# Softmax reciprocals stored as one row per head pair, and a new order of work where attention ends

## What is computed

```python
attn = np.exp(scores)
attn = attn / (np.sum(attn, axis=-1, keepdims=True) + 1e-09)
x = np.matmul(attn, v).transpose(0, 2, 1, 3).reshape(B * S, H * D)
h = x @ w_in
x = np.where(h > 0.0, h, np.exp(np.minimum(h, 0.0)) - 1.0) @ w_out
# then, per token: x + gate * (relu(x @ w1[e]) @ w2[e]) for its expert e, where x @ w_skip > 0
```

## Time and profile before

| | us |
|---|---|
| median of 3 runs | 791.72 |
| lowest and highest run | 790.86, 791.75 |
| the profiled execution | 791.72 |
| its span | 789.9 |

### The profile page before, as it was taken

How to read it: one execution, slowest core, us unless ns; L and a number is a source line. 1 busy time by engine, 2 the same in 40 slices (tenths; PEclk the granted TensorE clock), 3 DMA queues, 4 the chain that set the end, 5 groups by cost and what they waited for, 6 DMA issues and landing times.

```text
span 789.9 us, 15565 instructions
## 1 busy us (share of the span) xinstructions
PE 758.0 (96%) x5170; PEld 639.8 (81%) x5171; DVE 524.1 (66%) x1331; ACT 347.8 (44%) x830; POOL 245.3 (31%) x240
## 2 busy tenths in 40 slices
PE   5999999899999999999999999999987999999995
PEld 3777777688998888898988998888865777887884
DVE  3888888954337974984797598436665997367342
ACT  3888888644322213223222322324452774446231
POOL 4888887944501201210121021000112231222211
PEclk9999999999999999999999999999998999999998
DMA  9556677462422112101210200502424898174000
GB/s 163 133 149 157 163 162 188 144 198 61 147 79 103 48 57 91 50 21 62 59 41 0 90 22 27 214 0 81 135 95 126 270 340 303 46 229 153 34 15 9
DMA packets 101061, 88.15 MB, mean 112 GB/s; under 512 B 63812, under 2 KB 78532, under 8 KB 100880
## 3 DMA queue, kind: packets, MB, share of 16 engines
q1 hardware_dynamic: 95584, 81.89, 34.7%
q0 software_dynamic: 3056, 5.00, 1.9%
q10 hardware_dynamic: 2368, 0.59, 0.4%
HBM read 72.26 MB, written 18.34 MB: 115 GB/s over the span
## 4 chain that ended last, share of the span: by engine, by line
PE 86%; ACT 5%; DVE 4%; issue 3%; DVEq 1%; DMA 1%; POOL 0%; SPq 0%; ACTq 0%; POOLq 0%
PE h_ps L1733 12%; PE out_ps L1733 12%; PE h_ps L1734 12%; PE h_ps L1735 12%; PE out_ps L1735 11%; PE out_ps L1734 11%; PE o_ps L684 5%; PE s_ps L668 3%; ACT prob L541 3%; PE t_ps L593 2%; PE out_ps L1869 1%; PE s_ps L663 1%; ACT pt L525 1%; PE tr_ps L1834 1%; DMA raw_qk<-in_q_dram 1%
## 5 line engine op out<-in xcount | busy, mean ns | idle before, releaser
L1558 ACT ACTIVATE ex<-h_ps 128x384 f32<-128x384 f32 x96 | 47.3, 493 | 272.3 <-PE h_ps L1735 272.3
L1733 PE MATMUL h_ps<-xt_hi,wi_hi 128*128 128x384 f32 x384 | 131.8, 343 | 0.0
L1734 PE MATMUL h_ps<-xt_lo,wi_hi 128*128 128x384 f32 x384 | 129.7, 338 | 0.0
L1735 PE MATMUL h_ps<-xt_hi,wi_lo 128*128 128x384 f32 x384 | 129.7, 338 | 0.0
L1394 DVE TENSOR_SCALAR ex<-ex 128x384 f32<-128x384 f32 x96 | 36.9, 385 | 131.1 <-ACT ex L1558 129.7
L1733 PE MATMUL out_ps<-wo_hi,gt 128*128 128x512 f32 x288 | 114.5, 398 | 0.0
L1735 PE MATMUL out_ps<-wo_hi,gt 128*128 128x512 f32 x288 | 113.9, 396 | 0.0
L1734 PE MATMUL out_ps<-wo_lo,gt 128*128 128x512 f32 x288 | 113.3, 393 | 0.0
L541 ACT ACTIVATE prob<-s_ps,negmax 128x128 f32<-128x128 f32 (+2 forms) x144 | 77.8, 556 | 14.1 <-DVE negmax L399 13.7
L1276 DVE CUSTOM_DVE_ANT_0 x2t<-x,w_raw 128x512 bf16<-128x512 f32 x108 | 82.7, 806 | 0.4
L1172 POOL TENSOR_TENSOR xt_lo<-x_raw,xt_hi 128x384 fp32r<-128x384 f32 x20 | 28.3, 1413 | 157.8 <-ACT xt_hi L1575 157.5
(11 more groups left out here) (180 smaller groups left out, 1589.0 us busy)
## 6 DMA issues: line engine op xcount, KB each, us to landing
w_raw<-in_moe_w_dram SPq DMA_DIRECT2D x56, 512.0 KB, 5.2
raw_qk<-in_q_dram SPq DMA_DIRECT2D x32, 144.0 KB, 3.2
attn_t<-attn_sb SPq DMA_DIRECT2D x16, 288.0 KB, 2.2
x_raw<-attn_t SPq DMA_DIRECT2D x24, 192.0 KB, 2.4
w_raw<-recip_rows SPq DMA_DIRECT2D x48, 96.0 KB, 2.8
out_dram<-x SPq DMA_DIRECT2D x18, 256.0 KB, 2.1
x_rows<-x SPq DMA_DIRECT2D x18, 256.0 KB, 2.6
v<-in_v_dram SPq DMA_DIRECT2D x32, 128.0 KB, 2.9
```

The source lines that it names most:

```text
L1558: act.activation(ex[:, f % 2], h_ps[:, f % 2, 0:NB], ACT.Exp).then_inc(ex_done, 1)
L1733: pe.matmul(dst, stat[0], mov[0], start=start, stop=False, skip_group_check=True)
L1734: pe.matmul(dst, stat[0], mov[1], start=False, stop=False, skip_group_check=True)
L1735: return pe.matmul(dst, stat[1], mov[0], start=False, stop=stop, skip_group_check=True)
```

## The change

The table becomes 16 rows of 1152 numbers, one row for each pair, and a pair is stored with one DMA (`store_recips`). A block of 384 tokens no longer lies in one piece of that table: per batch the first 512 tokens and the last 64 are apart, for each of the two heads. A new generator gives the pieces, and `load_recips` issues a DMA for each: 2 for a tile of blocks 0 and 3, 6 for one of blocks 1 and 4 (widths 128, 64 and 192 for each half), 4 for one of blocks 2 and 5. The semaphore counts follow.

Further, the reciprocals of block 1 are loaded by `load_r(1, k)`, after the x tiles of block 1 and ahead of the gates and w_out's chunks 8 to 15. The x tile 3 of block 0 and its reciprocals are loaded one step later. At the end of attention SP stores the reciprocals of pair 15 ahead of the result of pair 14, DVE copies the result of pair 14 after its reciprocals of pair 15, and PE does `values(14)` after `turn_mixed` and `turn_recips(15)` ahead of hidden(1).

```diff
+def recip_row(r_rows, b, k):
+    PAIR_TOKENS, MAIN = 576, 512
+    for batch in range(4):
+        first = batch * PAIR_TOKENS
+        for a, z, at in ((0, MAIN, 0), (MAIN, PAIR_TOKENS, 2 * MAIN)):
+            lo, hi = max(first + a, b * X_TILES * P), min(first + z, (b + 1) * X_TILES * P)
+            if lo < hi:
+                for h in range(2):
+                    col = at + h * (z - a) + lo - first - a
+                    yield (slice(h * P // 2, (h + 1) * P // 2), slice(lo - b * X_TILES * P, hi - b * X_TILES * P),
+                           r_rows[4 * batch + k:4 * batch + k + 1, col:col + hi - lo]
+                           .broadcast_to([P // 2, hi - lo]))
...
+    for rows, cols, src in recip_row(r_rows, b, k):
+        sp.dma_start(dst[rows, cols], src).then_inc(x_r_in[min(b, 2)][k], 16)
...
         def store_recips(n, i):
             wait(sp, r_row_done, n + 1)
-            rows, first = bass.ds((n % GROUP) * 2, 2), (n // GROUP) * S
-            sp.dma_start(r_all[rows, bass.ds(first, FULL * P)].rearrange("h (u q) -> h u q", q=P),
-                         r_rows[0:2 * FULL, :]).then_inc(r_stored, 16)
-            sp.dma_start(r_all[rows, bass.ds(first + FULL * P, TAIL)].rearrange("(o h) q -> o h q", o=1),
-                         r_rows[2 * FULL:COLS, :].rearrange("o (h q) -> o h q", h=2)).then_inc(r_stored, 16)
+            sp.dma_start(r_all[bass.ds(n, 1)].rearrange("o (c q) -> (o c) q", q=P), r_rows[:, :])\
+              .then_inc(r_stored, 16)
...
-            for c in ((0, 1), (2, 3), (), ())[m - PAIRS + 4]:
+            for c in {PAIRS - 4: (0, 1), PAIRS - 3: (2,), PAIRS - 2: (3,), PAIRS - 1: ()}[m]:
                 load_x_rows(sp, attn_t, c, 0, x_raw, x_in)
                 load_recips(sp, r_all, 0, c, x_r[0][c], x_r_in)
-            for c in ((), (), (0, 1), (2, 3))[m - PAIRS + 4]:
-                load_recips(sp, r_all, 1, c, x_r[1][c], x_r_in)
         sp.wait_ge(s_done, SCORES * (PAIRS - 1))
         first_wo()
+        store_recips(PAIRS - 1, 1)
         store(PAIRS - 2, 0)
-        store_recips(PAIRS - 1, 1)
         next_wo()
         store(PAIRS - 1, 1)
...
-            if older and not now:
-                final(*older)
             if past:
                 recips(past[0])
...
-            if older and now:
+            if older:
                 final(*older)
...
-        values(*older, (t1_out, PAIRS))
         turn_tile(PAIRS - 1, 3, t_ps, t3_done, (exp_done, exps(PAIRS - 1, 3, 1)), (t2_out, PAIRS))
         pe.wait_ge(wi_lo_done, PAIRS)
         hidden(0)
         pe.wait_ge(t3_out, PAIRS)
         turn_mixed(last, None)
+        values(*older, (t1_out, PAIRS))
+        turn_recips(PAIRS - 1)
         hidden(1)
-        turn_recips(PAIRS - 1)
         values(*last, (corner_out, PAIRS), (t3_out, PAIRS))
...
             load_x(1)
+            for k in range(KC):
+                load_r(1, k)
             load_gates()
             for f in range(2 * WR, FC):
                 load_wo(f)
```

More of the change, by code:

```diff
@@ L64, in attention, with recip_loads, normalise @@
     given.update(q=q, k=k, v=v, w_in=w_in)
-def load_recips(sp, r_rows, b, k, dst, x_r_in):
[L70 to L76, removed]
+def recip_row(r_rows, b, k):
[10 more added lines that the diff above has]
+                           .broadcast_to([P // 2, hi - lo]))
+def load_recips(sp, r_rows, b, k, dst, x_r_in):
+    for rows, cols, src in recip_row(r_rows, b, k):
+        sp.dma_start(dst[rows, cols], src).then_inc(x_r_in[min(b, 2)][k], 16)
+def recip_loads(r_rows, b, k):
+    return sum(1 for b1 in range(min(b, 2), b + 1) for _ in recip_row(r_rows, b1, k))
+def normalise(dve, x, r, x_in, x_r_in, x_norm, b, k, loads):
     dve.wait_ge(x_in[k], 16 * (b + 1))
-    dve.wait_ge(x_r_in[min(b, 2)][k], 32 * (max(b, 2) - 1))
+    dve.wait_ge(x_r_in[min(b, 2)][k], 16 * loads)
     dve.tensor_tensor(x[k][:, :], x[k][:, :], r, ALU.mult).then_inc(x_norm, 1)
@@ L315, in sync @@
             sp.wait_ge(stored[i], 16 * (GROUP // 2))
-        sp.wait_ge(r_stored, 32 * 2 * GROUP)
+        sp.wait_ge(r_stored, 16 * GROUP)
         for m in range(PAIRS - 4, PAIRS):
             step(m // 2, m % 2)
-            for c in ((0, 1), (2, 3), (), ())[m - PAIRS + 4]:
+            for c in {PAIRS - 4: (0, 1), PAIRS - 3: (2,), PAIRS - 2: (3,), PAIRS - 1: ()}[m]:
                 load_x_rows(sp, attn_t, c, 0, x_raw, x_in)
                 load_recips(sp, r_all, 0, c, x_r[0][c], x_r_in)
-            for c in ((), (), (0, 1), (2, 3))[m - PAIRS + 4]:
-                load_recips(sp, r_all, 1, c, x_r[1][c], x_r_in)
         sp.wait_ge(s_done, SCORES * (PAIRS - 1))
         first_wo()
+        store_recips(PAIRS - 1, 1)
         store(PAIRS - 2, 0)
-        store_recips(PAIRS - 1, 1)
         next_wo()
@@ L433, in recip_rows @@
             wait(dve, r_turned, n + 1)
-            wait(dve, r_stored, 32 * n)
+            wait(dve, r_stored, 16 * n)
             dve.tensor_copy(r_rows[:, :].rearrange("c (s w) -> c s w", s=2), t_ps[0:COLS, :, 0:D])\
@@ L493, in vector @@
             for c in {PAIRS - 2: (0, 1), PAIRS - 1: (2, 3), PAIRS: ()}[m]:
-                normalise(dve, x_raw, x_r[0][c], x_in, x_r_in, x_norm, 0, c)
+                normalise(dve, x_raw, x_r[0][c], x_in, x_r_in, x_norm, 0, c, recip_loads(r_all, 0, c))
             step(m // 2, m % 2)
@@ L802, in experts @@
         x_hi_done, x_lo_done = sem("x_hi_done"), sem("x_lo_done")
-        r_all = nc.dram_tensor("recip_rows", (2 * KC, N), F32, kind="Internal").ap()
+        r_all = nc.dram_tensor("recip_rows", (N // (TB * P) * 8 // 3, 9 * P), F32, kind="Internal").ap()
         x_r_in, x_norm = [[sem(f"x_r_in{b}_{k}") for k in range(KC)] for b in range(3)], sem("x_norm")
@@ L1039, in load_r @@
             def load_r(b, k):
-                if (b, k) > (2, 0):
+                if b > 1 and (b, k) > (2, 0):
                     sp.wait_ge(x_norm, KC * b + k)
@@ L1094, in _ @@
                 sp.wait_ge(stored, 16 * attend["pairs"] // 2)
-            sp.wait_ge(attend["r_stored"], 32 * attend["pairs"])
+            sp.wait_ge(attend["r_stored"], 16 * attend["pairs"])
             load_x(1)
+            for k in range(KC):
+                load_r(1, k)
             load_gates()
@@ L1404, in step @@
                     k = X_AT.index(f + 1)
-                    normalise(dve, x_raw, x_r[b + 1][k], xr_in, x_r_in, x_norm, b + 1, k)
+                    normalise(dve, x_raw, x_r[b + 1][k], xr_in, x_r_in, x_norm, b + 1, k,
+                              recip_loads(r_all, b + 1, k))
                 if b == 0 and f == WR:
```

## The result

The changed kernel takes 801.68 us (median of four, 800.59 to 802.54), the kernel before, on the same chip and in turn with it, 791.29 us (790.39 to 791.75): a ratio of 1.0132 [1.0113, 1.0150], 10.4 us slower. The forecast was 798.2 us with a range up to 801.5. The profiled execution of the changed kernel took 800.32 us, with a span of 798.6 us against 789.9.

The account below looks back on a forecast made before the run. PE was taken as the bound, busy 96% of the span. Attention's 1.9 us delay lies inside the 6.5 us at chunk 5's output product, the other terms are 0: 791.72 + 6.5 = 798.2 us, range 794.2 to 801.5.

Parts of the forecast that it names:

- Step 1: Attention's steady part: one store of a pair's reciprocals in place of two saves SP about 0.7 us, worth 0.
- step 5: Later blocks: more reciprocal loads, six needing 6.3 us of the 8.4 available, worth 0.
- Step 2: End of attention: PE idles between tiles 2 and 3 of pair 15 until DVE has copied tile 2, +1.3 us.
- Step 3: End of attention: DVE waits for block 0's later x tile 3 reciprocals, delaying PE, +0.6 us (none to 1.2).
- the gain that I held possible: Tile 3's multiplication, run later and alone, may be faster and end up to 0.5 us earlier.
- Step 4: 24 loads delay w_out's chunk 8; PE stalls 4.6 us before chunk 5's output product, 6.5 us late including earlier delay.
- The price of an issue: SP's time per narrow load behind attention: 0.62 us taken; 0.50 gives a sum of 3.6 us, 0.69 gives 8.2.
- The cover of tile 0 of block 1: DVE's multiplication for that tile, delayed by six loads, is still in time for PE, by 0.4 us only.
- the sum: Whole kernel: 6.5 us slower, 798.2 us, main forecast with chance 0.50.
- rival 1: Behind the 4.6 us gap half clock costs 2.4 us more: 8.9 us slower, 800.6 us; chance 0.30.
- Rival 2: The 24 issues are cheap or overlap, chunk 8 is in time, no stall: 793.6 us; chance 0.15.
- Rival 3: Attention's steady part: one store less frees DVE and ACT, removing PE's 2.5 us wait: 791.1 us; chance 0.05.

Follow-up runs that it names:

- b12: Kernel before plus the new table with one store a pair and 24 loads for block 1, the last 12 behind w_out's chunks 8 to 11: 790.77 us, 1.0008.
- d21: Changed kernel with the last 3 of the 24 loads moved behind w_out's chunks 8 to 11: 797.04 us, ratio 1.0087.
- d18: Changed kernel with the last 6 of the 24 loads moved behind w_out's chunks 8 to 11: 793.69 us, ratio 1.0038.
- warm: Changed kernel plus 20 unused matmuls on PE in the gap ahead of chunk 5's output product in block 0: 798.13 us, ratio 1.0099.
- s3_fill2: Kernel before with x tile 3 of block 0 loaded one step later and two repeats of overwritten products filling PE's wait: 792.69 us, ratio 1.0032.

## Why the prediction was wrong, step by step

**Step 1** (one store, 0) and **step 5** (later blocks, 0): right in their sum, by b12 at 1.0008.

**Step 2** (+1.3): right. The gap is 1.28 us, and alone it costs 1.2.

**Step 3** (+0.6, at most 1.2): mis-sized. DVE waited 1.76 us for the DMA, where 0.6 were forecast. Half a microsecond of the difference is the load: the store ahead of it took 1.20 us for the 0.44 that I borrowed from another row, and DVE could begin at 149.34 and not at 148.8. The other half is DVE itself, which was ready at 147.6 and not at 148.14; I had taken for granted that it comes when it came in the trace before. The multiplication took 1.39 us, as before (the pair of the earlier trace rows ends at 149.50, the second begins at 148.14: 1.36), so the gain that I held possible did not come. PE waits 1.64 + 0.62 us where it waited 0.43, 1.8 us more. It had come 0.7 us ahead until then (it begins the products of pair 13 at 148.05 against 148.73) and is 1.2 us behind after it; by the comparisons the step costs 3 to 4 us of time.

**Step 4** (PE at 196.9, a gap of 4.6): right within 0.3 us in the place (197.12) and 0.6 in the gap (4.01, since PE arrived later by step 3). The mechanism is the one forecast, but that the place fits so closely is in part luck: against the forecast the 24 loads began 0.4 us sooner (174.8 for 175.2) and took 0.7 longer, the gates took 0.2 longer, and chunk 8 was there 2.8 us after its issue and not 3.2. The price of an issue, 0.62, was 0.65. The cover of tile 0 of block 1 held: DVE waits 2.26 us for its loads and PE does not notice.

**The clock.** This is the step that failed: the sum gave a gap of 4.6 us no price beyond its length, and rival 1, which did, got 0.30 against 0.50. Behind the gap of 4.01 us the runs show half clock for 6 us, 2.8 us lost. I let it down because the one place with half clock in the trace before had more idle time in all. That was a reason for doubt and none for preferring zero. The half clock came in all six profiles with a gap of 2.4 us or more in this layer, and cost 2.8 us in that of the changed kernel, close to the 2.4 that rival 1 worked out from those rows.

The reading of the earlier trace rows was also incomplete. The trace before has another gap, just ahead of those rows, and behind it the clock stays at 1.00 (timeline of PE, and a window):

```profile
589.03 0.47 PE L1733 MATMUL out_ps<-wo_hi,ht_hi 128*128 128x512 f32 x1 [2.50 <-DVE ht_lo L1466]
...
590.00:592.00 2.00, 2.00 (x10) 1.59 (x9) 0.79 (x6) 0.95 (x1) 0.21 (x1) 1.00 0.00 0
```

In the changed kernel the same gap is followed by half clock:

```profile
598.50 0.47 PE L1748 MATMUL out_ps<-wo_hi,ht_hi 128*128 128x512 f32 x1 [2.50 <-DVE ht_lo L1481]
...
600.00:602.00 2.00, 2.00 (x6) 1.59 (x5) 1.07 (x8) 0.41 (x1) 0.20 (x1) 0.50 0.00 0
```

All 19 profiles have this gap of 2.5 us, with the same instructions around it. In 13 the clock is 0.50 within 2.5 us behind it, in six it is not. So for gaps of this length the price is a matter of chance from one execution to the next. The rule of the Trainium skill (TensorE: Matmul & The Clock Gate, What's actually happening) named beside rival 1, half clock after idling, held for the gap of 4.0 us; behind the one of 2.5 us it came in some executions only.

**The sum.** In the profiled execution PE is 6.7 us late at chunk 5's product, 2.8 more behind the half clock, and 0.8 of that is given back by the end: 8.7 us on the span, where 6.5 were forecast and 8.9 by rival 1. The measured 10.4 us are 1.8 more than the 8.6 between the two profiled executions: the median of the changed kernel is 1.4 us above its profiled execution, and that of the kernel before 0.4 below its own. What the 1.4 are is not shown. The other four executions have a clock of 0.985 or 0.986 where this one has 0.988, but the mean clock does not follow the time of single executions, as said above. By the mean clocks 4.3 of the 10.4 us would be clock (0.0054 x 790, an estimate, with 0.9916 for the kernel before in the other comparisons). The same estimate gives 4.0 us for the two profiled executions (0.993 - 0.988), where the timeline shows 2.8. The range's upper end, 801.5, held rival 1 with dearer issues, but no larger step 3 and no more clock than its 2.4 us; the median lies 0.2 us above it.

**Rival 2** (cheap issues) is excluded: 15.64 us for 24. The rule of the Trainium skill that the prediction named with it (DMA: Bandwidth & Descriptors, Issuing engines are not separate DMA queues) does not hold for these narrow loads: each lands 2.5 us after its issue and takes 0.65 of SP to issue, so that a run of 24 costs six landings. **Rival 3** (DVE freed in the steady part) did not show: b12, with the single store, is no faster.

## What to carry to other kernels

Count DMAs of a queue, not their bytes, and ask what stands behind them: here the last six of 24 loads of 0.65 us ahead of one chunk of weights made 7.4 us, and in b12, with twelve of them behind that chunk and steps 2 and 3 left out, nothing was left to measure. Where a forecast has TensorE idle for some microseconds between full stretches, price the half clock behind it in the main case; a slow stretch of the trace itself gives its size, and more than one profile tells how often it comes. And of a step moved into a new neighbourhood, take the durations from that place, and ask whether the engine that waits will come sooner as well: a store borrowed from a quieter row was off by 0.8 us, and DVE's arrival by 0.6.

## What the runs showed of the hardware that I had not expected

- A gap of 2.4 us on PE was followed by half clock in d21, one of 2.5 us where the experts begin in 13 of 19 profiles, and one of 1.1 us behind a full stretch was not (d18). Waits of 1.6 and 0.6 us brought it in the profiles of d21 and d18, but not in those of the changed kernel and of warm, which have the same waits. Behind the stall it lasted from 3 to 6 us with gaps between 3.7 and 5.1 us, and not in their order.
- Two multiplications of 128x384 took 2.85 us in the kernel before and 1.00 in the changed one, in the same place:

```profile
137.57 1.00 DVE L100 TENSOR_TENSOR x_raw<-x_raw,w_raw 128x384 f32<-128x384 f32 x2
```

  All twelve profiles with one store a pair have 1.0 there, the seven with two stores 2.1 to 2.9. In the trace of before they run beside work of POOL, and in that of the changed kernel POOL is idle from 137.3 to 138.3; that this is the cause was not tested. In the two profiles where they took longest (before 2.85, s3_fill2 2.72) PE waits 0.8 and 0.6 us soon after, in the other five with two stores 0.2 us at most. In the medians no gain shows (b12).
- The one store of 9x128 takes SP 0.31 to 0.52 us in the changed kernel; the two of before took 1.41 together. Here, too, the number of DMAs counts.
